# Attention in column tiles, the own term on TensorE, packed counts in the later routing searches, and weight splits moved

## What is computed

```
for t in range(S):                       # attention, r k v: [4, 8, 768, 48]
    cur = (u * k[t]) outer v[t]
    y[t] = r[t] @ (state + cur)
    state = w * state + k[t] outer v[t]
x = y as [3072, 384]
logits = x @ w_gate                      # [3072, 8]
order = argsort(-logits.flatten())       # greedy: each token to one expert, 384 tokens per expert
out[mask_e] = relu(x[mask_e] @ w1[e]) @ w2[e]        # w1 [384,1024], w2 [1024,384]
h = relu(out @ w_in);  y = (h * h) @ w_out           # w_in [384,2048], w_out [2048,384]
```

## Time and profile before

| | |
|---|---|
| median of 3 runs | 871.23 (870.90 to 871.38) |
| the profiled execution's own time | 872.39 |
| its span, first to last instruction | 870.7 |
| mean granted TensorE clock, of full speed | 0.966 |
| busy PE / DVE / ACT / POOL | 812.3 / 549.3 / 317.3 / 301.0 |
| attention | about 14 to 162.5 |
| first routing | 162.5 to 205 |
| experts | 206 to the end |

### The profile page before, as it was taken

The page is one execution under the profiler, slowest core; times in us unless marked ns, Lnnn a source line. Parts: engine busy times, 40 slices in busy tenths (PEclk is TensorE's granted clock), DMA queues, the critical chain, the costliest instruction groups (busy, mean ns, idle before and its releaser), DMA issues.

```text
span 870.7 us, 18546 instructions
## 1 busy us (share of the span) xinstructions
PE 812.3 (93%) x6695; PEld 778.8 (89%) x6695; DVE 549.3 (63%) x1223; ACT 317.3 (36%) x693; POOL 301.0 (35%) x288
## 2 busy tenths in 40 slices
PE   5999999525999999999999999999999999999995
PEld 3999999415899999999999999999999999999995
DVE  7899999585586469456935782677458534931210
ACT  1454554212154315422542353135315432532332
POOL 6555655012035205420531153126303520541232
PEclk9999999756999999999999999999999999999998
DMA  8688876022012003100400130022001200400000
GB/s 225 205 245 245 248 235 185 20 75 98 2 73 100 28 0 105 66 27 0 168 3 27 48 123 0 27 72 99 21 6 72 99 27 1 174 1 28 2 1 27
DMA packets 22144, 69.86 MB, mean 80 GB/s; under 512 B 3552, under 2 KB 6752, under 8 KB 22112
## 3 DMA queue, kind: packets, MB, share of 16 engines
q1 hardware_dynamic: 19040, 59.99, 21.7%
q0 software_dynamic: 3072, 9.44, 3.1%
HBM read 59.98 MB, written 9.44 MB: 80 GB/s over the span
## 4 chain that ended last, share of the span: by engine, by line
PE 75%; DVE 4%; issue 1%; POOL 1%; ACT 1%; DMA 0%; DVEq 0%; ACTq 0%; POOLq 0%
PE bank L1190 16%; PE bank L1191 15%; PE bank L1192 15%; PE bank L1244 8%; PE bank L1245 8%; PE bank L1246 8%; PE bank L1137 3%; DVE hot L796 1%; PE bank L1170 1%; DVE hot L885 1%; PE bank L1159 1%; POOL xg L428 0%; DMA xg<-x_rows,perm_next 0%; POOL out L464 0%; PE bank L1143 0%
## 5 line engine op out<-in xcount | busy, mean ns | idle before, releaser
L456 POOL TENSOR_TENSOR h_lo<-sq,h_hi 128x384 fp32r<-128x384 f32 x128 | 152.9, 1197 | 398.8 <-DVE sq L960 398.7
L960 DVE SCALAR_TENSOR_TENSOR sq<-bank,relu 128x384 f32<-128x384 f32 x128 | 70.9, 554 | 133.5 <-ACT relu L554 133.2
L554 ACT ACTIVATE relu<-bank 128x384 f32<-128x384 f32 x128 | 63.1, 493 | 198.8 <-PE bank L1192 196.6
L1244 PE MATMUL bank<-m_hi,h_hi 128*128 128x384 f32 x384 | 131.9, 344 | 0.0
L1190 PE MATMUL bank<-x_hi,m_hi 128*128 128x384 f32 x384 | 130.4, 340 | 0.3
L1246 PE MATMUL bank<-m_hi,h_lo 128*128 128x384 f32 x384 | 129.6, 338 | 0.0
L1245 PE MATMUL bank<-m_lo,h_hi 128*128 128x384 f32 x384 | 129.4, 337 | 0.0
L1191 PE MATMUL bank<-x_lo,m_hi 128*128 128x384 f32 x384 | 129.1, 336 | 0.0
L1192 PE MATMUL bank<-x_hi,m_lo 128*128 128x384 f32 x384 | 129.0, 336 | 0.0
L548 ACT ACTIVATE h_hi<-bank 128x384 fp32r<-128x384 f32 x64 | 31.5, 493 | 192.4 <-PE bank L1192 192.4
L952 DVE SCALAR_TENSOR_TENSOR h_lo<-bank,h_hi 128x384 fp32r<-128x384 f32 x64 | 35.5, 554 | 71.8 <-ACT h_hi L548 71.8
(11 more groups left out here) (172 smaller groups left out, 1569.5 us busy)
## 6 DMA issues: line engine op xcount, KB each, us to landing
w_raw<-we_in SPq DMA_DIRECT2D x48, 512.0 KB, 4.4
nn<-nn_in SPq DMA_DIRECT2D x24, 576.0 KB, 4.6
tt<-tt_in SPq DMA_DIRECT2D x48, 192.0 KB, 5.1
m_raw<-m_in SPq DMA_DIRECT2D x12, 512.0 KB, 5.6
x_rows<-yrow SPq DMA_DIRECT2D x24, 192.0 KB, 2.4
xg<-x_rows,perm_next POOLq DMA_INDIRECT x24, 4.6
out<-xg,perm_now POOLq DMA_INDIRECT x24, 2.6
u_row<-u_in SPq DMA_DIRECT2D x1, 192.0 KB, 5.7
```

Of the source, the lines that this page charges most:

```text
L456: pool.tensor_tensor(h_lo[g % 3][:, :], sq[g % 2][:, :], h_hi[g % 3][:, :].bitcast(f32), ALU.subtract).then_inc(lo2_ready, 1)
L554: act.activation(relu[:, :], h_ps[g % 3][:, 0:CAP], ACT.Relu).then_inc(relu_ready, 1)
L960: dve.scalar_tensor_tensor(out=sq[g % 2][:, :], in0=h_ps[g % 3][:, 0:CAP], scalar=0.0, in1=relu[:, :], op0=ALU.max, op1=ALU.mult).then_inc ...
L1244: pe.matmul(acc_ps[t][:, 0:DM], h_hi[r][:, s], m2_hi[:, c:c + DM], start=first, stop=False)
```

## The change

In words, part by part:

1. **Column tiles.** `back` and `gate` cut each matmul in two, each with 64 weight columns that go to one half of the output partitions; in `back` the moving columns are cut from 128 to 64.
2. **Own term.** POOL multiplies r and k by head (`rk`, 112 x 512, from tt), PE multiplies that with `u_pair` (eight matmuls with 112 rows, 64 weight columns and 2 moving columns, `own_term`, behind `front`), ACT copies the 8 sums (`own_copy`). DVE's `own_sum` and POOL's `rku` go; nn no longer carries r. ACT's order in a unit is now own_copy(n+1), turned_y(n-1), own_values(n+1), gated(n-1).
3. **Filler** matmuls per unit: 2 for 4.
4. **Dense weights.** Only the six tiles of w_in are split during the attention (one per four units; the low half by POOL in four parts of 256 columns, in place over m2_raw). The six of w_out are loaded behind the attention, rounded by ACT during the first routing; their low halves are made by POOL (tiles 0 and 1, once all six tiles of the first expert's weights are split) and by DVE inside the first expert (g = 13, 16, 18, 21). `contract` waits for them.
5. **First expert's weights.** POOL splits none. DVE waits until POOL has issued the gather, splits tiles 0 to 2, makes the three x_lo, then splits tile 3.
6. **Packed counts.** In the six later searches the thresholds are 64, 32, 32 (upper half) and 32, 32, 64 (lower half), the units' compares lie side by side in `flat`, and one matmul has the 128 columns of 2 or 4 units as weights and 16 or 32 moving columns: 12 or 6 matmuls for 24. DVE then adds the 2 or 4 blocks of the result (`fold`), each waiting for the one before. The threshold step k = 0 has an instruction of its own now, in all searches. `add_full` moves one matmul later. The first search keeps 41 thresholds and 24 matmuls.

```diff
-FILL = 4
+FILL = 2
-T = 41
-STEPS = [T * T, T, 1]
+T = [[64, 32, 32], [32, 32, 64]]
+STEPS = [[1024, 32, 1], [2048, 64, 1]]
+OUT_EARLY = 2
+OUT_LOW_AT = {13: 2, 16: 3, 18: 4, 21: 5}
+        def out_low(eng, j):
+            eng.wait_ge(out_hi_ready, j + 1)
+            cols = slice((IN_TILES + j) * WT, (IN_TILES + j + 1) * WT)
+            return eng.tensor_tensor(m2_lo[:, cols], m2_raw[:, cols], m2_hi[:, cols].bitcast(f32), ALU.subtract)
...
                         sp.wait_ge(scaled, 4 * i + b + 1)
+                        sp.wait_ge(rk_ready, 4 * i + b + 1)
                         load_tt(b, 4 * i + b + 4)
...
+            for j in range(OUT_TILES):
+                sp.dma_start(m2_raw[:, (IN_TILES + j) * WT:(IN_TILES + j + 1) * WT], m2_d[IN_TILES + j, :, :]).then_inc(out_loaded[j], 16)
             sp.wait_ge(logit_ready, NU)
             load_expert(0)
...
-            for j in range(POOL_TILES):
-                split_low(pool, 0, j)
             gather(0)
+            pool.sem_inc(gather_sent, 1)
             keep_perm(0)
+            pool.wait_ge(w_lo_ready, WE_TILES)
+            for j in range(OUT_EARLY):
+                out_low(pool, j).then_inc(out_lo_early, 1)
...
+            def in_low(i, part):
+                pool.wait_ge(in_hi_ready, i + 1)
+                cols = bass.ds(i * WT + part * (WT // B), WT // B)
+                pool.tensor_tensor(m2_lo[:, cols], m2_raw[:, cols], m2_hi[:, cols].bitcast(f32), ALU.subtract).then_inc(in_lo_ready, 1)
...
+                    did(f"fold{half}{k}0", dve.tensor_copy(folded[0:t, :], cnt_ps[0:t, 0:E]))
+                    for j in range(1, P // t):
+                        after(f"fold{half}{k}{j - 1}")
+                        did(f"fold{half}{k}{j}", dve.tensor_tensor(folded[0:t, :], cnt_ps[j * t:(j + 1) * t, j * E:(j + 1) * E],
+                                                                   folded[0:t, :], ALU.add))
...
-            dve.wait_ge(w_lo_ready, POOL_TILES)
-            for j in range(POOL_TILES, W1_TILES + 1):
+            dve.wait_ge(gather_sent, 1)
+            for j in range(W1_TILES):
                 split_low(dve, 0, j)
             for d in range(DC):
                 x_low(0, d)
+            split_low(dve, 0, W1_TILES)
...
+                        if is_first(i) and g in OUT_LOW_AT:
+                            out_low(dve, OUT_LOW_AT[g]).then_inc(out_lo_ready, 1)
                         if W_AT < g <= W_AT + WE_TILES:
                             split_low(dve, i + 1, g - W_AT - 1)
...
-                        last = pe.matmul(y_ps[j][:, a, p * P:(p + 1) * P], am[j][:, a, p * P:(p + 1) * P],
-                                         nn[b][:, :, :].rearrange("p x f -> p (x f)")[:, c.start:c.start + P],
-                                         start=False, stop=p == PAIRS - 1)
+                        for t in range(0, P, HALF):
+                            last = pe.matmul(y_ps[j][t:t + HALF, a, p * P:p * P + HALF], am[j][:, a, p * P + t:p * P + t + HALF],
+                                             nn[b][:, :, :].rearrange("p x f -> p (x f)")[:, c.start:c.start + HALF],
+                                             start=False, stop=p == PAIRS - 1)
...
+            def own_term(n, j):
+                pe.wait_ge(rk_ready, n + 1)
...
+                for p in range(PAIRS):
+                    for t in range(0, P, HALF):
+                        last = pe.matmul(own_ps[t:t + HALF, 2 * p:2 * p + 2], rk[j][:, p, t:t + HALF], u_pair[:, p, :],
+                                         start=True, stop=True)
+                last.then_inc(own_made, 1)
...
-                    last = pe.matmul(lg_ps, yT[:, d * P:(d + 1) * P], wg[:, d, :], start=d == 0, stop=d == DC - 1)
+                    for t in range(0, P, HALF):
+                        last = pe.matmul(lg_ps[t:t + HALF, :], yT[:, d * P + t:d * P + t + HALF], wg[:, d, :],
+                                         start=d == 0, stop=d == DC - 1)
...
+                many = P // T[half][k]
+                for a in range(0, NU, many):
...
+                    pe.matmul(cnt_ps[:, 0:many * E], flat[:, a * T[half][k]:a * T[half][k] + P],
+                              openc[:, a:a + many, :].rearrange("p u e -> p (u e)"), start=a == 0, stop=False)
```

More of the change, by code:

```diff
@@ L72, in _route_names @@
         for k in range(3):
-            names += [f"thr{half}{k}"] if k else []
-            names += [f"ge{half}{k}a", f"ge{half}{k}b", f"full{half}{k}", f"base{half}{k}"]
+            names += [f"thr{half}{k}", f"ge{half}{k}a", f"ge{half}{k}b"]
+            names += [f"fold{half}{k}{j}" for j in range(P // T[half][k])]
+            names += [f"full{half}{k}", f"base{half}{k}"]
     names += ["at_least", "reached", "reached_sum",
@@ L133, in build @@
         kn = sb("kn", [P, DM], f32, att)
-        rk = sb("rk", [P, DM], f32, att)
-        rku = [sb(f"rku{j}", [P, DM], f32, att) for j in range(2)]
+        rk = [sb(f"rk{j}", [HD, PAIRS, P], f32, att) for j in range(2)]
         own = [sb(f"own{j}", [P, H], f32, att) for j in range(2)]
@@ L150, in build @@
         zeros = sb("zeros", [HD, P], f32, att)
-        u_row = sb("u_row", [P, DM], f32, att)
+        u_pair = sb("u_pair", [HD, PAIRS, 2], f32, att)
         wg = sb("wg", [P, DC, E], f32, att)
-        m2_raw = [sb(f"m2_raw{j}", [P, WT], f32, att) for j in range(2)]
         att.close()
@@ L367, in _ @@
             pool.iota(part_id[:, :], [[0, 1]], base=0, channel_multiplier=1, **iota).then_inc(made, 1)
-            for k in range(3):
-                last = pool.iota(steps[:, k, :], [[STEPS[k], T]], base=0, channel_multiplier=0, **iota)
-            last.then_inc(made, 1)
+            pool.iota(ramp[:, :], [[1, 64]], base=0, channel_multiplier=0, **iota).then_inc(made, 1)
             pool.memset(held_m[:, :, :], 0.0)
@@ L596, in _ @@
             dve.memset(w_s[:, :], 1.0).then_inc(w_gap, 1)
+            dve.memset(u_pair[:, :, :], 0.0).then_inc(u_gap, 1)
             for b in range(2):
@@ L688, in units @@
                     rows(i, b)
-                    if not last or b < B - 1:
-                        own_sum(*one)
                     if not last:
                         state_sum(*one)
-                    m2_low(i, b)
             tabbed()
@@ L1018, in _ @@
                 split_low(dve, 0, j)
-            with dve.Fori(0, E - 2) as i:
+            expert(0, False, True)
+            with dve.Fori(1, E - 2) as i:
                 expert(i, False, True)
@@ L1109, in units @@
                         front(i + (b + 1) // B, (b + 1) % B)
+                    if not end:
+                        own_term(n + 1, (b + 1) % 2)
                     if not is_first(n):
@@ L1186, in _, with three @@
                         last.then_inc(x_sum, 1)
-            def three(out, hi_w, lo_w, hi_x, lo_x, first, last):
+            def three(out, hi_w, lo_w, hi_x, lo_x, first, last, between=None):
                 pe.matmul(out, hi_w, hi_x, start=first, stop=False)
+                if between:
+                    between()
                 pe.matmul(out, hi_w, lo_x, start=False, stop=False)
```

210 lines of the change are left out of this document (124 added, 86 removed).

## The result

The changed kernel takes 875.66 us in the median of six executions, against 870.92 for the kernel before beside it: ratio 1.005, 95% interval 1.0036 to 1.0065. Five of the six lie between 874.24 and 878.91 and give the ratio; the sixth, 889.11, is a slow one and is left out of it (the median of the five is 875.52). The change makes the kernel slower by half a per cent, where 855.3 and a range of 845 to 867 were forecast. The profiled execution took 875.80, its span is 874.1.

What follows compares the result with a forecast made beforehand. Attention bound by PE with DVE just behind, first routing by a DVE, POOL and DMA chain, experts by PE. 872.39 - 15.2 - 0.3 + 5.5 - 6.6 + 0.7 = 856.5; less 1.16, 855.3 us; range 845 to 867.

Steps and rivals of the forecast that it cites:

- Back, gate, own term, filler: Attention unit on PE: 64-column records at 33 ns, two fillers fewer saving 0.21; unit 5.17 us instead of 5.86.
- a late start: Attention's start: POOL's 512-wide product delays DVE's ks by about 0.7 us, against about 0.7 early at the end.
- 22 periods x 0.69 = -15.2: Whole attention: each of 22 unit periods gains 0.69 us, -15.2 in all; ends -21 and +15.
- a rival in which they lock `rs`: Attention bound by DVE's mask-ks-rs loop under POOL's locks, or drains: unit 5.7, gain 3.5, total 867; chance 0.15.
- First routing: Stretch between attention and experts: dropping POOL's weight split brings x_hi slightly forward, -0.3 us; ends -3 and +1.
- The lock at the first expert: First expert: POOL's two output splits block DVE's pick 4.4 us, plus 1.1 for lower clock; +5.5, gap 5.6.
- the half clock: First expert: nine matmuls behind the blocked pick run at a lower clock, about 1.1 us.
- DVE's output splits: First expert: DVE's four w_out splits delay perm and the gather ahead of h_lo, +0.7 us; ends 0 and +3.
- Packed counts: Six later searches: fewer matmuls save 2.50 us, delays cost 1.4, so 1.1 gained each, -6.6; ends -15 and 0.
- The lower half's first count: Later searches: a fourth small step ahead of the lower half's first compare makes the count's second half 0.35 late.
- their 0.2: Later searches: DVE's folds make add_full 0.05 us late, four times, 0.2 per search.
- The sign named for it: Later searches: the forecast is wrong if PE's idle in a search is far from 1.4 us.

Runs made afterwards that it cites:

- e6_gate: e4_all with DVE's go-ahead to split weights signalled by a small POOL write behind the gather descriptors instead of an increment: 850.73 us, one execution.
- e5_fill: e4_all with 13 more filler matmuls ahead of the second attention unit's scores, in PE's idle near 20 us: 848.61 us, ratio 0.9741 to before.
- e1_paced: The changed kernel with POOL's three m_lo products of the last pass made behind the pass and DVE's scales: 865.91 us, ratio 0.9936 to before.
- e4_all: The changed kernel with POOL's last-pass m_lo late, both early output splits on DVE, and DVE's expert loop written out: 852.53 us, 0.9774 to before.

## Why the prediction was wrong

- **Back, gate, own term, filler: right.** Unit 5.19 for 5.17, records at 31 ns for 33, two fillers at 0.22 for 0.21. With nothing in its way the attention ends 16.2 earlier than before (146.26), where 15.2 were forecast. That the two are so near is in part luck: 22 periods give 15.0, of which 1.0 is half clock that before had in its second period (6.82 for 5.86; its four versions with idle increments show none there in their profiles, and their first `best` comes at 160.90 to 161.47), and 1.3 lie behind the last scores, which the sum had set off against a late start that did not come.
- **"22 periods x 0.69 = -15.2" failed.** It took the last pass for one like the others. The prediction had POOL's three products beside DVE's loop, and even a rival in which they lock `rs`, but in every unit; it never asked what paces POOL where `kn` falls away. There `rk` and `m_lo` run beside `rs`, which takes 2.5 longer, PE idles 2.20, and the half clock makes 9.6 of it. Another 2.7 went at the start, to half clock behind an idle that the kernel before had too (1.46 for 1.68; its clock was down for 3.4 us, here for 6.9). So the attention gave 3.9 and not 15.2.
- **First routing: right by luck.** -0.27 for -0.3, but with the increment overtaking the descriptors, which stayed at 1.15 to 1.97. In the order the prediction assumed (e6_gate) it is +1.2 or so, beyond the +1 of its upper end. Nor was tile 3 the last to come: its rounding had ended (199.11 and 1.06) when `x_hi` still waited for PE, which turns the gathered rows:

```profile
201.43 1.25 ACT L577 ACTIVATE x_hi<-bank 128x384 fp32r<-128x384 f32 x3 [1.26 <-PE bank L1262]
```

- **The lock at the first expert: right in kind and place, too high in size.** Idle 5.40 for 5.6. The stretch rose by 3.06 for 5.1. Of 4.4 more idle 4.17 came (5.40 less 1.23), and the packed counts give 1.43 back; that leaves 0.3 for the half clock (213.8 to 220.6) and DVE's output splits together, which were priced at 1.1 and 0.7. No run measured the two apart. Undoing it gives 3.15.
- **Packed counts: gain right and a little low, its parts only in part.** 1.43 a search for 1.1, so they cost 1.07 where 1.4 was priced. The lower half's first count is 0.36 late, as forecast (0.35). The folds made `add_full` of the earlier steps no later than 1.35, so their 0.2 did not come; the first count lost 0.28 where 0.1 was priced. The sign named for it, an idle of PE near 1.4 a search, is not there: 0.46 shows as idle, the rest stands inside the counts.
- **What the sum did not have at all:** 11.7 for DVE's backward jump, the second step that failed. The prediction counted what the folds cost in time, never what they and the register work add to the loop body (227 to 271 instructions), nor that moving expert 0 out of the loop and into straight code shifts the loop from 317 to 454. No row of before shows such a stop, since its loop does not stop at the jump; the Trainium skill's section named above would have raised the question.

Without 9.6 + 2.7 and 11.7, the profile's 875.8 would be 851.8, inside the range; with the 3.15 of the lock gone too 848.6 (e5_fill: 848.61). That the last two agree to a tenth is chance, as the half clock differs from profile to profile.

The best version found, e5_fill, is 2.6% under the kernel before: the change as it is, with POOL paced in the last pass, no output splits of POOL, DVE's loop written out and one idle filled. A shift by some thirty idle instructions in place of writing out should do as well; it was tried alone, not with the other edits, which move the loop by a few instructions too.

## To carry to other kernels

Price a steady loop and then walk its last pass: an engine that was paced by a wait that ends with the loop will run at once, and whatever it locks is paid at the worst place, since here one PE gap of 2.2 us was followed by half the clock for the rest of the stage. Count what an edit adds to a hardware loop's body, and look at the instruction queue's packets before and after: if they grow by more than the code, as here (33 for 11), look for a stop at the loop's jump; here a shift of 30 instructions, or straight code, took it away. When totals scatter by more than the effect, compare stretches between two events that every version has.

## What the runs showed of the hardware beyond what was expected

- A backward jump on DVE is followed by a stop of 2.4 to 3.2 us for a loop of 271 instructions at 454, 582 or 710 of its program, and by none at 484; nor for one of 275 at 317 or of 227 at 454. That it is a matter of 128-instruction pieces is inferred.
- An increment on POOL's queue behind three indirect DMAs takes effect before the second and third have been issued (DVE started at 194.40, they at 194.88 and 196.75); a small write with an increment waits for them.
- An idle of PE of 1.68 us near 20 us was followed by nothing (e1_paced), by 6.9 us (the changed kernel) or by 13.7 us (e4_all) at half clock in profiles with the same work up to there; one of 2.20 ahead of 135 by half clock to the end of the stage, one of 0.83 (e1_paced) by none.
- DVE's `rs` beside POOL's `rk` takes 1.76 where alone it takes 0.68, and in e1_paced this costs PE 0.83 at most.
